# Attention with VectorE two units ahead instead of three, its loads in another order, and three edits around it

## What is computed

```python
def _attn_ref(q, k, v, alpha) -> np.ndarray:      # each (4, 8, 768, 48)
    state = np.zeros((B, H, D, D), dtype=np.float32)
    for t in range(S):
        state = alpha[:, :, t, :, None] * state + np.einsum('bhd,bhe->bhde', k[:, :, t], v[:, :, t])
        y[:, :, t] = np.einsum('bhd,bhde->bhe', q[:, :, t], state)

def reference(**kwargs):
    attn_out = _attn_ref(**attn_kwargs)
    x = np.ascontiguousarray(attn_out.transpose(0, 2, 1, 3)).reshape(B * S, H * D)
    x = _moe_ref(x=x, **moe_kwargs)       # 8 experts: logits = x @ w_gate, a greedy choice with 384 tokens each, relu MLP
    return _moe2_ref(x=x, **moe2_kwargs)  # silu(x @ w_gate) * (x @ w_val) @ w_out, the same weights for all tokens
```

## Time and profile before

| | before |
|---|---|
| median of 3 executions | 913.92 us (912.94 to 914.73) |
| the profiled execution: its own time | 914.68 us |
| its span, first to last instruction | 912.9 us |
| TensorE busy over the span | 853.5 us (94%) |
| VectorE busy over the span | 512.2 us (56%) |
| TensorE's mean granted clock | 0.966 of full speed |
| first cut of the routing (L740) | at 148.94 us |

### The profile page before, as it was taken

How to read it: one execution, slowest core, us unless ns; L and a number is a source line. 1 busy time by engine, 2 the same in 40 slices (tenths; PEclk the granted TensorE clock), 3 DMA queues, 4 the chain that set the end, 5 groups by cost and what they waited for, 6 DMA issues and landing times.

```text
span 912.9 us, 17432 instructions
## 1 busy us (share of the span) xinstructions
PE 853.5 (94%) x6582; PEld 801.4 (88%) x6582; DVE 512.2 (56%) x1057; ACT 280.4 (31%) x505; POOL 253.2 (28%) x200
## 2 busy tenths in 40 slices
PE   6999996699969999999999999999999999999991
PEld 4788874399869999999999999999999999999991
DVE  6999985637824464457445634664365536533330
ACT  1344441223214232422332332333233332333210
POOL 2322210165944023403240414050305130522001
PEclk8999997699979999999999999999999999999996
DMA  8789960400310022003200410030013002300000
GB/s 333 267 331 334 337 220 35 153 13 23 100 43 26 0 91 72 27 0 103 60 26 0 129 42 18 20 127 26 17 63 101 17 9 69 95 26 1 1 1 29
DMA packets 25858, 77.27 MB, mean 85 GB/s; under 512 B 3808, under 2 KB 10464, under 8 KB 22880
## 3 DMA queue, kind: packets, MB, share of 16 engines
q1 hardware_dynamic: 22752, 67.39, 21.2%
q0 software_dynamic: 3072, 9.44, 3.3%
HBM read 67.38 MB, written 9.44 MB: 84 GB/s over the span
## 4 chain that ended last, share of the span: by engine, by line
PE 74%; POOL 3%; DVE 2%; issue 1%; DMA 1%; ACT 0%; POOLq 0%; ACTq 0%
PE ps_up L1572 44%; PE ps_acc L1572 26%; PE ps_turn L818 2%; POOL gated_low L1231 2%; POOL w_low L1375 1%; PE ps_turn L1578 1%; PE ps_turn L838 0%; PE ps_turn L823 0%; DVE quick_at_row L794 0%; DMA x_tok<-x_rows,slot_token 0%; DMA x_tok<-x_rows,from_rows 0%; DVE quick_over_cut L740 0%; POOL out L1397 0%; PE ps_up L1578 0%; POOL x_tok L1369 0%
## 5 line engine op out<-in xcount | busy, mean ns | idle before, releaser
L1375 POOL TENSOR_TENSOR w_low<-w_raw,w_high 128x768 fp32r<-128x768 f32 x60 | 130.3, 2178 | 256.3 <-ACT w_high L1463 255.9
L1572 PE MATMUL ps_up<-z_high,gated_high 128*128 128x384 f32 x576 | 197.5, 343 | 0.2 <-DVE z_low L1530 0.2
L1572 PE MATMUL ps_up<-z_high,gated_low 128*128 128x384 f32 x576 | 195.7, 340 | 0.0
L1572 PE MATMUL ps_up<-z_low,gated_high 128*128 128x384 f32 x576 | 194.0, 337 | 0.0
L1572 PEld LDWEIGHTS ps_up<-z_high,gated_high 128*128 128x128 f32 x576 | 108.7, 189 | 0.9 <-issue 0.5
L1572 PEld LDWEIGHTS ps_up<-z_low,gated_high 128*128 128x128 f32 x576 | 108.7, 189 | 0.0
L1572 PEld LDWEIGHTS ps_up<-z_high,gated_low 128*128 128x128 f32 x576 | 108.6, 189 | 0.0
L1535 DVE TENSOR_TENSOR act_out<-ps_up,act_out 128x384 f32<-128x384 f32 x96 | 53.5, 558 | 94.5 <-ACT act_out L1479 92.7
L1482 ACT CAST u_high<-act_out 128x384 fp32r<-128x384 f32 x96 | 49.2, 513 | 170.5 <-DVE act_out L1539 170.5
L1572 PE MATMUL ps_acc<-gated_high,u_high 128*128 128x384 f32 x288 | 97.5, 339 | 1.8 <-DVE u_low L1542 1.8
L1572 PE MATMUL ps_acc<-gated_high,u_low 128*128 128x384 f32 x288 | 96.8, 336 | 0.0
(11 more groups left out here) (164 smaller groups left out, 1433.0 us busy)
## 6 DMA issues: line engine op xcount, KB each, us to landing
w_raw<-in_experts SPq DMA_DIRECT2D x64, 384.0 KB, 3.1
qka_in<-in_qka SPq DMA_DIRECT2D x23, 1026.0 KB, 8.4
gated_raw<-in_gated SPq DMA_DIRECT2D x12, 576.0 KB, 6.6
v_in<-in_v SPq DMA_DIRECT2D x24, 192.0 KB, 8.3
x_rows<-y_rows SPq DMA_DIRECT2D x24, 192.0 KB, 5.0
qka_in<-in_qka SPq DMA_DIRECT2D x1, 512.0 KB, 5.5
out<-o_tok,to_rows POOLq DMA_INDIRECT x24, 2.6
x_tok<-x_rows,from_rows POOLq DMA_INDIRECT x21, 3.2
```

Source lines behind the costliest of these rows:

```text
L1375: pool.tensor_tensor(w.low[:, m % RING, :], w.raw[:, m % RING, :], w.high[:, m % RING, :].bitcast(F32), ALU.subtract).then_inc(w_low_ready, 1)
L1572: mm = pe.matmul(acc, lhs[a], rhs[b], start=(first and i == 0), stop=(last and i == 2))
```

## The change

1. VectorE works on `decays`/`undecays` of 0 and 1 ahead of the loop; in turn u it now does `decays(u + 2)`, `mask_scores` of u, `advance` of u-1, `undecays(u + 2)`.
2. SP's order at the start is new: unit 1's block in two pieces, the decays first, with a semaphore of their own (`alpha1_in`); the identity and the mask ahead of unit 2's block; the turner (gate weights) behind the first values, with its own semaphore; unit 3's block ahead of the other values, unit 4's ahead of the constants and the first shared weights. In the loop SP loads unit u+5 and not u+6.
3. TensorE no longer waits for identity and turner before the first front, and issues `fill` matmuls (L427's) behind the first two fronts: 8 and 10.
4. In the last chunk ScalarE rounds no pieces of the shared weights; it does so at the head of the next stage.
5. The transpose of the extremes (`turn_ends`) moves ahead of the last `outputs`, the spread (`spread_ends`) ahead of the last turn. That turn writes to the keys' bank (`ps_k`), so that it doesn't wait for the copy of the logits before it, and its logits are copied ahead of its rows.

```diff
@@ SP, the start @@
-            load(1)
-            sp.dma_start(idt[:], ident).then_inc(consts_in, 16)
-            sp.dma_start(turner[:], turn_gate).then_inc(consts_in, 16)
+            sp.dma_start(qka_in[1][:, ALPHA_AT:QKA], qka[1, :, ALPHA_AT:QKA]).then_inc(alpha1_in, 16)
+            sp.dma_start(qka_in[1][:, 0:ALPHA_AT], qka[1, :, 0:ALPHA_AT]).then_inc(qka_loaded[1], 16)
+            sp.dma_start(idt[:], ident).then_inc(idt_in, 16)
             sp.dma_start(mask[:], causal).then_inc(mask_in, 16)
+            load(2)
             load_v(0, 0)
-            load(2)
-            for b in range(1, B):
-                load_v(b, b)
-            quick.load(sp, consts)
-            for r in range(2):
-                w.load_gated(sp, 0, r)
+            sp.dma_start(turner[:], turn_gate).then_inc(turner_in, 16)
...
-            for u in range(BUFFERS, 6):
-                load_next(u)
+            load_next(3)
+            for b in range(1, B):
+                load_v(b, b)
+            load_next(4)
+            quick.load(sp, consts)
+            for r in range(2):
+                w.load_gated(sp, 0, r)
             for i in range(CH):
                 for j in range(B):
                     u, b, c = unit(i, j)
-                    if u + 6 < UNITS:
-                        load_next(u + 6)
+                    if u + 5 < UNITS:
+                        load_next(u + 5)
@@ VectorE @@
-            for u in range(3):
+            for u in range(2):
                 decays(u)
                 undecays(u)
-            dve.wait_ge(mask_in, 16)
             for u in range(UNITS):
+                if u + 2 < UNITS:
+                    decays(u + 2)
                 if u == 0:
-                    mask_scores(0, 0)
-                if u + 3 < UNITS:
-                    decays(u + 3)
-                if u + 1 < UNITS:
-                    mask_scores((u + 1) // B, (u + 1) % B)
-                if u + 3 < UNITS:
-                    undecays(u + 3)
-                if u <= UNITS - B:
-                    advance(u // B, u % B)
+                    dve.wait_ge(mask_in, 16)
+                mask_scores(u // B, u % B)
+                if 1 <= u <= UNITS - B + 1:
+                    advance((u - 1) // B, (u - 1) % B)
+                if u + 2 < UNITS:
+                    undecays(u + 2)
@@ ScalarE, the last chunk @@
-                step(CH - 1, j, ahead=False, split_after={0: 0, 1: 1})
-            y_copy(CH - 1, B - 1)
-            lg_copy(CH - 1, B - 1)
+                step(CH - 1, j, ahead=False, split_after={})
+            act.wait_ge(y_turned, UNITS)
+            lg_copy(CH - 1, B - 1, last_turned_out)
+            y_copy(CH - 1, B - 1, last_turned_out)
@@ TensorE @@
             pe.wait_ge(zeroed, 2)
-            for n in range(WARMUPS):
-                pe.matmul(ps_y_cols[:, 0:512], warm[:, 0, 0:P], warm, start=True, stop=True)
-            pe.wait_ge(consts_in, 16 * 2)
-            front(0, 0, started=False)
-            front(0, 1, started=False)
+            fill(WARMUPS)
+            for j in range(2):
+                front(0, j, started=False)
+                fill(FILL[j])
...
             for j in range(B):
+                if j == B - 1:
+                    pe.wait_ge(state_ready, UNITS - B + 1)
+                    quick.turn_ends(pe)
                 step(CH - 1, j, ahead=(j < 2), keys=False, updated=(j == 0))
-            pe.wait_ge(state_ready, UNITS - B + 1)
-            quick.begin_tensor(pe)
+            quick.spread_ends(pe)
             pe.wait_ge(y_cols_copied, UNITS)
-            pe.wait_ge(lg_copied, UNITS - 1)
-            gate_and_turn(CH - 1, B - 1)
+
+            pe.wait_ge(k_tok_ready, UNITS - B + 2)
+            gate_and_turn(CH - 1, B - 1, last_turned_out)
@@ ScalarE, the next stage @@
             with start(act):
+                if not again:
+                    for r in range(2):
+                        w.split_gated_high(act, CH - 1, r)
                 for m in range(RING):
                     split_high(0, m)
```

More of the change, by code:

```diff
@@ L30 @@
 WARMUPS = 22
+FILL = (8, 10)
 WARM_TURNS = 20
@@ L81, in attention @@
         ps_y_rows = ps("ps_y_rows")
-        y_turned_out = ps_y_rows[:, 0:PAIRS * TURN_N].rearrange("p (a n) -> p a n", a=PAIRS)
-        consts_in = sem("consts_in")
+        y_turned_out, last_turned_out = (bank[:, 0:PAIRS * TURN_N].rearrange("p (a n) -> p a n", a=PAIRS)
+                                         for bank in (ps_y_rows, ps_k))
+        idt_in = sem("idt_in")
+        turner_in = sem("turner_in")
         zeroed = sem("zeroed")
@@ L90, in attention @@
         qk0_in = sem("qk0_in")
+        alpha1_in = sem("alpha1_in")
         v_loaded = [sem(f"v_loaded{b}") for b in range(B)]
@@ L193, in decays @@
                     dve.wait_ge(alpha0_in, 16)
+                elif u == 1:
+                    dve.wait_ge(alpha1_in, 16)
                 else:
@@ L219, in undecays @@
                     dve.wait_ge(qk0_in, 16)
+                if u == 1:
+                    dve.wait_ge(qka_loaded[1], 16)
                 dve.tensor_tensor(k_und[u % 2][:], part(u, 1), k_und[u % 2][:], ALU.mult).then_inc(k_ready, 1)
@@ L283, in scale_q @@
                     pool.wait_ge(qk0_in, 16)
+                if u == 1:
+                    pool.wait_ge(qka_loaded[1], 16)
                 pool.tensor_tensor(q_dec[u % B][:], part(u, 0), decay[u % B][:, :, 1:SEG], ALU.mult).then_inc(q_ready, 1)
@@ L305, in y_cols_copy, with y_copy @@
                 act.copy(y_cols[j % 2][:], ps_y_cols[:, :]).then_inc(y_cols_copied, 1)
-            def y_copy(i, j):
+            def y_copy(i, j, of=y_turned_out):
                 u, b, c = unit(i, j)
@@ L362, in front @@
                         pe.wait_ge(k_tok_ready, u)
+                    else:
+                        pe.wait_ge(idt_in, 16)
                     for a in range(PAIRS):
@@ L397, in update, with gate_and_turn @@
                 mm.then_inc(update_ready, 1)
-            def gate_and_turn(i, j):
+            def gate_and_turn(i, j, into=y_turned_out):
                 for a in range(PAIRS):
-                    mm = pe.matmul(y_turned_out[:, a, :], y_cols[j % 2][:, a * P:(a + 1) * P], turner[:, a, :],
+                    mm = pe.matmul(into[:, a, :], y_cols[j % 2][:, a * P:(a + 1) * P], turner[:, a, :],
                                    start=True, stop=True)
@@ L419, in step @@
                         pe.wait_ge(lg_copied, u - 1)
+                    else:
+                        pe.wait_ge(turner_in, 16)
                     gate_and_turn(i, j - 1)
@@ L422, in step, with fill @@
                     front(i, j + 2, keys=keys)
+            def fill(count):
+                for n in range(count):
+                    pe.matmul(ps_y_cols[:, 0:512], warm[:, 0, 0:P], warm, start=True, stop=True)
             pe.wait_ge(zeroed, 2)
-            for n in range(WARMUPS):
-                pe.matmul(ps_y_cols[:, 0:512], warm[:, 0, 0:P], warm, start=True, stop=True)
-            pe.wait_ge(consts_in, 16 * 2)
-            front(0, 0, started=False)
-            front(0, 1, started=False)
+            fill(WARMUPS)
+            for j in range(2):
+                front(0, j, started=False)
+                fill(FILL[j])
             for j in range(B):
@@ L680, in spread_cuts, with turn_ends @@
         link(dve.tensor_copy(self.base[:], self.low[:]))
-    def begin_tensor(self, pe):
+    def turn_ends(self, pe):
         pe.wait_ge(self.ready, self.SET)
@@ L685, in begin_tensor, with spread_ends @@
         pe.transpose(self.bank[0:2, 0:P], self.ends[:], self.idt[:]).then_inc(self.ends_turned, 1)
+    def spread_ends(self, pe):
         pe.wait_ge(self.end_ready, 1)
```

6 lines of the change are left out of this document (3 added, 3 removed).

## The result

| | before | after |
|---|---|---|
| median of 20 executions each | 913.9 us (912.58 to 915.35) | 920.25 us (914.36 to 927.77) |
| ratio | | 1.0069, 95% interval 1.0051 to 1.0086 |
| the profiled execution's own time, span | 914.68, 912.9 | 921.14, 917.8 |
| own time less span | 1.8 | 3.3 |
| mean granted clock | 0.966 | 0.968 |

What follows compares the result with a forecast made beforehand. It took the attention's start as bound by arriving blocks and VectorE, its middle by TensorE, its tail by a chain of waits. Terms -4.7 + 5.0 - 2.8 = -2.5 from the median 913.92 gave 911.4 us, range 906.0 to 917.0.

Steps and rivals of the forecast that it cites:

- The start: Start of the attention: earlier blocks and scans bring the first full TensorE step to 35.7 from 40.40, minus 4.7 us.
- The late blocks: Middle of the attention: blocks of units 9, 13, 17, 21 land 1.25 us late each, plus 5.0 us, bounds 3.2 and 6.4.
- The clock falls in the new holes: Rival, middle: low clock behind TensorE's new holes, a further 1.7 us a chunk, adding 6.8, to 918.2 us; chance 0.07.
- The tail: End of the attention: hidden weight splits and reordered last operations, minus 2.8 us, bounds minus 1.3 (low clock) and minus 3.2.
- Cost nothing: Start: the 18 fill matmuls, 3.8 us in all, delay nothing, since outputs and update still finish before VectorE needs them.
- a fixed chain: Behind the attention: routing and experts move as a block with what the attention wins or loses, with no term of their own.

Runs made afterwards that it cites:

- e3_no_fill: The changed kernel without its 18 fill matmuls (FILL = (0, 0)); ratio to before 1.0037.
- e2_tail_alone: The kernel before with only the tail's edits (parts 4 and 5 of the change); 913.82 us, ratio to before 0.9995.
- e11_fill_the_holes: The changed kernel with 6 more fill matmuls ahead of the outputs of each looping chunk's last unit; 915.92 us, ratio to before 1.0024.
- e1_block_ahead: The changed kernel with SP loading block u+6 again instead of u+5, ahead of the store; 909.63 us, ratio to before 0.9952.
- e5_no_fill: e1_block_ahead without the 18 fill matmuls; ratio to before 0.9945.
- e6_fewer_warmups: e1_block_ahead with 4 warm-ups instead of 22, fills unchanged; 909.04 us in one execution.
- e9_both: e1_block_ahead with the transpose of the ends behind the last outputs and no fills; 905.86 us, ratio to before 0.9915.
- e4_start_alone: The kernel before with only the start's edits (parts 2 and 3), block u+6 and VectorE three units ahead kept; 914.46 us, ratio to before 1.0005.
- e7_block_before_pair: The changed kernel with SP loading the block ahead of the pair of shared weights, still u+5; 912.5 us, ratio to before 0.9984.
- e8_ends_late: e1_block_ahead with the transpose of the ends behind the last outputs instead of ahead; 906.93 us, ratio to before 0.9926.
- e10_40_warmups: The kernel before with 40 warm-ups instead of 22 and nothing else; 918.08 us in one execution.
- e12_half_the_fills: e1_block_ahead with 4 and 5 fill matmuls instead of 8 and 10; 906.69 us in one execution.

## Why the prediction was wrong

- **The start** (forecast -4.7) was right: -4.83. Unit 1's scan started at 8.31 (8.5), unit 2's at 12.74 (12.85), unit 3's at 17.14 (17.45), and the first full step at 35.57 (35.7).
- **The late blocks** (forecast +5.0, four of 1.25) were right in place and, in the profiled execution, in their sum: 1.51, 1.21, 1.81 and 0.43, 4.96 together. That the sum comes out so close is in part luck, since the single holes lie far from 1.25, and in `e3_no_fill` the same four sum to 6.25. The blocks of those places landed in 8.3, 8.8, 9.3 and 8.0 us, around the 8.4 and 9.2 that I took. The rule by which they would have landed in an estimated 4.4 us (the Trainium skill, DMA: Bandwidth & Descriptors, Anatomy of one DMA) again doesn't hold in this queue: 5.6 is the least of 22.
- **"The clock falls in the new holes", chance 0.07, is the step that failed.** My reason was that the only hole with a low clock behind it was of 1.80 us, and "mine are shorter". My own bounds had one hole at up to 1.6, the measured ones reach 1.81, and one row of before can't say below what length it is safe. It cost 4.64 us in the profiled execution from one fall, where I had 1.7 for a fall, 6.8 for four: the low clock of before held for some 3.5 us, this one for the 10.3 from 100.70 to 111.00. In the median it cost some 3 us. It doesn't happen in each execution alike (the mean clock of the 20 runs from 0.961 to 0.973): I needed a chance for each hole, not one for all.
- **The tail** (forecast -2.8, bound -1.3 with the low clock) came at -1.2 in the profiled execution. It is the bound: the clock fell behind the wait of 1.43 (forecast 1.35), and the last turn came 9.81 us after unit 22's outputs, not 8.1. In the eight other kernels that have this wait (1.42 to 1.44) it did not bring the low clock in the profiled execution, and in `e2_tail_alone` the tail was 2.9 shorter, as forecast.
- **"Cost nothing" for the fills** held for the path on the engines, and failed in a place that my sum didn't have: 1.5 us outside the span. That own time and span can differ was in the table I started from (914.68 and 912.9), and I took the difference for a constant.
- **Behind the first cut** I had "a fixed chain". The span shows +1.1 there in the one profile of after (765.1 us for 764.0). In the profiled executions of all fourteen kernels this stretch took 763.6 to 766.1 us, so 1.1 is within what it varies by; the cause is open.

From the forecast of -2.5 to the profiled execution's +6.46 these are 8.9 of 8.96: 4.64 for the clock in the middle, 1.6 for the tail, 1.5 outside the span, 1.1 behind the first cut, and 0.1 between start and middle. The forecast had the holes; it lacked what follows a hole.

This account is of one execution, and the medians are less well explained. The tail's edits alone gained 0.7 us in the median and not 2.8, and the start's alone 1.7 in the median of the spans, where its profiled execution had the first full step 2.9 sooner. And the median span of `e11_fill_the_holes` is 2.6 above before's, that of `e1_block_ahead` 6.0 below: 8.6 us for late blocks with little or no loss of clock, where in the two profiled executions the way from the first full step to unit 22's outputs differs by only 5.6 (100.40 for 94.83). So +5.0 for the late blocks is shown for the profiled execution, and may be too small for the median; no run tells.

## What to carry to other kernels

A load's slack is counted from its place in the issuing queue to its consumer, with the landing time that the trace shows under load, and a change that shortens the consumer's lead has to be matched by the loader's: here one unit of distance was worth 10.6 us. A hole on TensorE in a stretch that it bounds costs its length and, in some executions, a low clock behind it; so a shift of work that opens many short holes is to be priced as a spread, and a widened spread is the first sign of it. Compare the execution's own time with its span before and after, since a gain in the span can be lost outside it.

## What the runs showed of the hardware

The time outside the span falls into two groups, and the number of matmuls at the start goes with it, but not in proportion. It was 1.8 or 1.9 us in every execution of before and of the kernels with as many of these matmuls as it, 22 (`e2_tail_alone`, `e3_no_fill`, `e5_no_fill`, `e6_fewer_warmups` with 4 warm-ups and 18 fills, and `e9_both`), 2.9 to 3.7 in every execution of all six with 18 more (after, `e1_block_ahead`, `e4_start_alone`, `e7_block_before_pair`, `e8_ends_late`, `e10_40_warmups`), and again 1.8 with 9 more (`e12_half_the_fills`) and, in `e11_fill_the_holes`, with 24 more in the program, 42 executed. For the 18 it doesn't seem to depend on where they stand or on what they wait for: in the one execution of `e10_40_warmups` they are warm-ups ahead of everything. The length of TensorE's program, or how it is laid out, would fit; no run tells this apart, and the cause stays open.

The clock fell to 0.50 behind idle times of TensorE of 1.81 and 1.43 us in the profiled execution of after, and not behind those of 1.51 and 1.21 in the same one, nor behind 1.84 in `e3_no_fill`, where the windows show 1.00 afterwards. The widest pair stands in these two rows, the first of `e8_ends_late`, where the outputs take 1.89 us at the low clock (0.50 from 32.20 to 35.00), the second of `e4_start_alone`, where they take 1.08 at 1.00:

```profile
31.95 1.89 PE L391 MATMUL ps_y_cols<-scores,v_in 128*48 128x128 f32 x16 [1.46 <-DVE scores L237]
...
135.24 1.08 PE L391 MATMUL ps_y_cols<-scores,v_in 128*48 128x128 f32 x16 [2.88 <-ACT y_cols L316]
```

So the length of a hole doesn't settle it: 1.46 brought the low clock and 2.88 didn't, and the wait of 1.42 to 1.44 at the tail brought it in one of nine profiled executions.
